# Four PSUM banks for the last MLP, and tasks that take turns where one MLP follows another

## The reference, cut to what matters

```
scores = q @ k.T / 8                        # 32 heads of 64 columns, 576 rows
p = exp(scores - max) where scores >= max - tau, else 0
x = (p / sum(p)) @ v                        # rows: (batch, 576), columns: 8 heads x 64

u = x + (x.T @ U @ V).T                     # mix over the 576 rows, rank 32
z = u + relu(u @ w_ch1) @ w_ch2             # MLP, 512 -> 2048 -> 512

logits = z @ w_gate; keep = sigmoid(z @ w_local) >= 0.5
e = previous row's expert where keep, else argmax(logits)
out = softmax(logits)[e] * (relu(z @ w1[e]) @ w2[e])     # 8 experts, 512 -> 1024 -> 512
```

## Time and profile before

| what | value |
|---|---|
| median of 3 runs | 1099.58 us (1099.11 to 1101.6) |
| the profiled execution's own time | 1100.43 us |
| its span, first to last instruction | 1098.7 us |
| TensorE busy | 1050.1 us, 96% |
| VectorE, ScalarE, GpSimd busy | 513.9, 469.9, 370.6 us |
| TensorE in the chain that ended last | 82% of the span |

### The profile page before, as it was taken

One profiled execution on the slowest core, in us unless ns is written; L12 is line 12 of the kernel. 1 busy time (PEld: TensorE's weight loads), 2 busy tenths in 40 slices (PEclk: granted clock), 3 DMA queues, 4 the chain that ended last, 5 costly groups with the idle time before them and its releaser, 6 DMA issues.

```text
span 1098.7 us, 20001 instructions
## 1 busy us (share of the span) xinstructions
PE 1050.1 (96%) x7142; PEld 920.0 (84%) x7142; DVE 513.9 (47%) x1022; ACT 469.9 (43%) x914; POOL 370.6 (34%) x341
## 2 busy tenths in 40 slices
PE   6999899999989999998999999899989999999997
PEld 5666799999769989986999997899978888888885
DVE  4675554445444444444454443322275543254642
ACT  5776543444454344445434433322214433244531
POOL 5454222624501553441064334068501111121111
PEclk9999999999999999999999999999999999999999
DMA  7887151535251542616052322432056444154621
GB/s 166 188 183 188 39 126 55 138 92 130 93 130 36 144 115 85 160 49 174 12 147 67 93 76 72 145 134 78 1 198 201 137 134 159 39 200 133 211 75 41
DMA packets 110729, 127.52 MB, mean 116 GB/s; under 512 B 67229, under 2 KB 67229, under 8 KB 110624
## 3 DMA queue, kind: packets, MB, share of 16 engines
q1 hardware_dynamic: 104480, 114.54, 36.7%
q0 software_dynamic: 3600, 11.01, 3.1%
q10 hardware_dynamic: 2544, 0.59, 0.2%
HBM read 88.16 MB, written 10.22 MB: 90 GB/s over the span
## 4 chain that ended last, share of the span: by engine, by line
PE 82%; SPq 6%; ACT 3%; DVE 3%; issue 3%; DMA 2%; POOL 0%; POOLq 0%; ACTq 0%; DVEq 0%
PE mlp_banks L697 19%; PE mlp_banks L689 18%; PE p_down L1387 11%; PE p_up L1387 11%; PE aux L647 6%; PE score_banks L623 5%; PE score_banks L630 5%; PE p_turn L1414 2%; DMA mlp_rows<-z_rows 1%; PE aux L590 1%; PE p_x L1381 1%; DVE stat L939 1%; PE mlp_banks L672 1%; SPq L291 1%; ACT u_hi L843 1%
## 5 line engine op out<-in xcount | busy, mean ns | idle before, releaser
L794 ACT ACTIVATE ex<-score_banks,stat 128x576 f32<-128x576 f32 x132 | 97.8, 741 | 178.0 <-DVE stat L939 178.0
L469 POOL CAST w_hi<-stage 128x1024 fp32r<-128x1024 f32 x64 | 66.6, 1040 | 288.1 <-PE mlp_banks L689 240.4
L689 PE MATMUL mlp_banks<-u_hi,w_hi 128*128 128x320 f32 (+1 forms) x512 | 157.0, 307 | 3.7 <-ACT u_hi L843 3.3
L697 PE MATMUL mlp_banks<-hid_hi,w_hi 128*128 128x320 f32 (+1 forms) x512 | 158.5, 309 | 0.9 <-DVE hid_lo L987 0.9
L948 DVE SCALAR_TENSOR_TENSOR ex<-score_banks,stat,ex 128x576 f32<-128x576 f32 x132 | 107.7, 816 | 107.0 <-ACT stat L798 105.7
L474 POOL TENSOR_TENSOR w_lo<-stage,w_hi 128x1024 fp32r<-128x1024 f32 (+1 forms) x70 | 154.1, 2203 | 4.8
L689 PE MATMUL mlp_banks<-u_hi,w_lo 128*128 128x320 f32 (+1 forms) x512 | 151.4, 296 | 0.0
L697 PE MATMUL mlp_banks<-hid_lo,w_hi 128*128 128x320 f32 (+1 forms) x512 | 151.3, 296 | 0.0
L697 PE MATMUL mlp_banks<-hid_hi,w_lo 128*128 128x320 f32 (+1 forms) x512 | 151.3, 296 | 0.0
L689 PE MATMUL mlp_banks<-u_lo,w_hi 128*128 128x320 f32 (+1 forms) x512 | 151.3, 295 | 0.0
L987 DVE SCALAR_TENSOR_TENSOR hid_lo<-mlp_banks,hid_hi 128x256 fp32r<-128x256 f32 (+1 forms) x128 | 58.4, 456 | 113.5 <-ACT hid_hi L845 112.8
(11 more groups left out here) (237 smaller groups left out, 1812.6 us busy)
## 6 DMA issues: line engine op xcount, KB each, us to landing
stage<-in_moe_w_ch SPq DMA_DIRECT2D x64, 512.0 KB, 3.7
w_raw<-in_moe_w SPq DMA_DIRECT2D x64, 512.0 KB, 5.1
q_tiles<-q_parts SPq DMA_DIRECT2D x30, 320.0 KB, 3.9
q_tiles<-q_parts SPq DMA_DIRECT2D x60, 160.0 KB, 4.2
k_tiles<-k_parts SPq DMA_DIRECT2D x60, 144.0 KB, 3.4
raw_q<-in_q SPq DMA_DIRECT2D x32, 128.0 KB, 3.1
raw_v<-in_v SPq DMA_DIRECT2D x32, 128.0 KB, 2.9
raw_k<-in_k SPq DMA_DIRECT2D x28, 128.0 KB, 2.7
```

Source lines behind the costliest of these rows:

```text
L469: nc.gpsimd.tensor_copy(w_hi[:, n % RING], stage[:, n % 2]).then_inc(w_upper, 1)
L689: last = nc.tensor.matmul(bank[:, 0:w], ch1(a, g, d, c), of[:, d, cols], start=(d == 0 and n == 0), stop=(d == KC - 1 and n == 2))
L697: last = nc.tensor.matmul(bank[:, 0:w], ch2(a, g, q, c), of[:, q, 0:w], start=(q == 0 and n == 0), stop=(q == QUARTER - 1 and n == 2))
L794: nc.scalar.activation(ex_of(n), score_of(n), ACT.Exp, bias=stat[:, n % 4, 0:1], scale=-1.0).then_inc(exp_done, 1)
```

## The change

`mlp_tasks` writes the list in another order. `banks_of_tasks` gives the tasks of the last batch, from `token_mix` to the last `logits`, four banks in turn: the two of `mlp_banks` and the first half of each of the two `score_banks`, which attention has left by then. Elsewhere a task's bank is t % 2 as before. `LEFT_BY[t]` is the task that used the bank before t; TensorE waits for its evictions.

- Start of batches 0 to 2: `mixed` of block 0 in turn with what batch b-1 left; then that rest in turn with the first `hidden` of block 0; then the first `channel` of block 0 in turn with `mixed` of block 1. In batch 0 nothing is left from before, so block 0's `mixed` and `hidden` stand alone.
- End of batches 0 and 1: `gate`, `logits` and the two `rows` of block 0 in turn with the last `hidden` of block 1. Block 1's last `channel`, `gate`, `logits` and `rows` are what is left to the next batch.
- Batch 2 to 3: `token_mix`, two `rows`, `mixed` of block 0, three `rows`, `mixed` of block 1.
- `tasks_by_step` has other counts of tasks per step; again 237 stand in attention's steps.
- `g4` has a buffer of its own, since `token_mix` now stands between `hidden` and `channel`. The last row of batch 2 is copied to `o_cols`, and doesn't wait for a store. `gate` of block 1 waits for the stores of the two rows of block 0 before it writes over `z_rows`. `logits` waits on TensorE for its own `gate`.
- The stationary side of the gate's products has 16 columns for 32; that of `rows` and `turn_out` for the last 64 rows has 64 for 128. Two clears at the start are gone.

The core of the diff:

```diff
 def mlp_tasks():
-    tasks = []
+    tasks, left = [], []
     for b in range(B):
+        def quarter(kind, k, r):
+            return [(b, kind, k, r, c) for c in range(KC)]
+
         rows = [(b, "rows", 0 if i < BLOCKS[0][1] else 1, i, 0) for i in range(NT)]
+        gate, logits = ([(b, kind, k, 0, 0) for k in range(2)] for kind in ("gate", "logits"))
         tasks.append((b, "token_mix", 0, 0, 0))
-        if b:
-            tasks += waiting
-        tasks += [(b, "mixed", k, 0, c) for k in range(2) for c in range(KC)]
+        if b < B - 1:
+            tasks += taking_turns(left[:KC], quarter("mixed", 0, 0))
+            tasks += taking_turns(left[KC:], quarter("hidden", 0, 0))
+            tasks += taking_turns(quarter("channel", 0, 0), quarter("mixed", 1, 0))
+        else:
+            tasks += left[:SPLIT_ROWS] + quarter("mixed", 0, 0) + left[SPLIT_ROWS:] + quarter("mixed", 1, 0) + quarter("hidden", 0, 0) + quarter("channel", 0, 0)
         for r in range(NQ):
             for k in range(2):
-                tasks += [(b, "hidden", k, r, q) for q in range(QUARTER)]
-                tasks += [(b, "channel", k, r, c) for c in range(KC)]
-        tasks += [(b, "gate", k, 0, 0) for k in range(2)]
-        tasks += [(b, "logits", k, 0, 0) for k in range(2)]
-        tasks += rows[:SPLIT_ROWS]
-        waiting = rows[SPLIT_ROWS:]
-    return tasks + waiting
+                if (r, k) not in ((0, 0), (NQ - 1, 1)):
+                    tasks += quarter("hidden", k, r) + quarter("channel", k, r)
+        if b < B - 2:
+            tasks += taking_turns([gate[0], logits[0]] + rows[:BLOCKS[0][1]], quarter("hidden", 1, NQ - 1))
+            left = quarter("channel", 1, NQ - 1) + [gate[1], logits[1]] + rows[BLOCKS[0][1]:]
+        else:
+            tasks += quarter("hidden", 1, NQ - 1) + quarter("channel", 1, NQ - 1) + gate + logits
+            left = rows
+    return tasks + left
...
+def banks_of_tasks():
+    first, last = INDEX[B - 1, "token_mix", 0, 0, 0], INDEX[B - 1, "logits", 1, 0, 0]
+    bank, user, left_by = [], {}, []
+    for t in range(len(TASKS)):
+        n = t - first
+        bank.append(t % 2 + (2 if first <= t <= last and n % 4 >= 2 else 0))
+        left_by.append(user.get(bank[t]))
+        user[bank[t]] = t
+    return bank, left_by
...
         if b == 1:
-            want = 0 if at == 0 else 1 if at == 1 else 3 if at in (6, 15, 17, 26) else 2
+            want = min(at, 2)
...
-            else:
-                pe.wait_ge(act_task, emptied(BY_ACT, t - 2))
-                pe.wait_ge(dve_task, emptied(BY_DVE, t - 2))
-            bank = mlp_banks[:, 512 * (t % 2):512 * (t % 2) + 512]
+            elif LEFT_BY[t] is not None:
+                pe.wait_ge(act_task, emptied(BY_ACT, LEFT_BY[t]))
+                pe.wait_ge(dve_task, emptied(BY_DVE, LEFT_BY[t]))
+            bank = task_bank(t)
...
             elif kind == "logits":
+                pe.wait_ge(act_task, emptied(BY_ACT, INDEX[b, "gate", k, 0, 0]))
...
+                if k == 1 and b < B - 2:
+                    act.wait_ge(rows_stored[0], 16 * (3 * b + 1))
+                    act.wait_ge(rows_stored[1], 16 * (2 * b + 1))
...
-                if b < B - 1 and stored:
+                if b < B - 1 and stored and (b, r) != (B - 2, NT - 1):
                     act.wait_ge(rows_stored[r % 2], 16 * stored)
```

More of the change, by code:

```diff
@@ L96, in tasks_by_step @@
     assert done == INDEX[B - 2, "channel", 1, NQ - 1, KC - 1] + 1
+    for want in (3, 1):
+        plan.append(list(range(done, done + want)))
+        done += want
     while done < len(TASKS):
@@ L202, in attention_and_mlp, with task_bank @@
     aux = ctx.enter_context(nc.psum_tensor("aux", [P, 1024], F32))
+    def task_bank(t):
+        n = BANK_OF[t]
+        return mlp_banks[:, 512 * n:512 * n + 512] if n < 2 else score_banks[:, n - 2, 0:512]
     def bank_of(n):
@@ L709, in task @@
                 for d in range(KC):
-                    last = nc.tensor.transpose(bank[:, d * P:(d + 1) * P], z_at(k, d, n * P, P), ident[:])
+                    last = nc.tensor.transpose(bank[0:ROWS[r], d * P:(d + 1) * P], z_at(k, d, n * P, ROWS[r]), ident[:])
             last.then_inc(task_done, 1)
```

39 lines of the change are left out of this document (23 added, 16 removed).

## The result

The changed kernel took 1093.2 us (median of 5 runs, 1091.9 to 1094.66) where the kernel before took 1099.58 (by now of 5 runs, 1099.11 to 1101.6): a ratio of 0.9932, with a 95% interval of 0.9922 to 0.9943. It is faster by 6.4 us by the medians; the ratio would be 7.5. The forecast was a gain of 15.9 and a range that ended at 1092, so the sign was right and both the time and the range were wrong.

The account below looks back on a forecast made before the run. TensorE, busy 96% of the span, was taken as the bound, so only its idle or slow-clock time could be won. 6.9 + 5.4 + 0.4 + 3.9 + 0.5 = 17.1 off 1100.43 gave 1083.3, against the median 1084.1; forecast 1083.7, range 1078.5 to 1092.

Parts of the forecast that it names:

- Part 1: The two borders inside attention: of 10.1 and 8.6 us lost, 3.2 stay at each, so gains of 6.9 and 5.4.
- Two kinds of stall stay: At each border inside attention, a step's chain (six times 0.45, 2.7 us) and waits inside `gate` and `logits` (0.5) stay.
- Clock: At the first border inside attention, TensorE ran mostly at 1.2 GHz after idling 1.69 us; counted as 1.6 us to win.
- Part 2: Start of the first MLP: two waits go, 1.3 us come back in steps 42 to 45; gain 0.4, between -2.5 and 1.7.
- Part 3: Last border: the first `hidden` starts at 694.9 for 698.8, a gain of 3.9 us, at worst 1.5.
- Part 4: Inside the last MLP and its end: a gain of 0.5 us in all (0 to 1), 0.4 at the end.
- Part 5: Small edits: nothing from 16 gate columns for 32 (-0.5 to +0.5 us), the 64-column transposes or the two dropped memsets.
- A: Rival: stalls only spread; 15 steps with one large task each lose 1.0 us, not 0.45; 1092 us, chance 19%.
- The forecast's own sign of being wrong: A gain under 9 us, with many waits of 1 us on the copies of turned scores, would make the forecast wrong.
- B: Rival: light steps borrow from fuller ones on both sides, 0.45 becomes 0.15 us; 5 us more, 1079, chance 11%.
- C: Rival: SP and GpSimd come late, the pair's stacking misses step 80; 2 x 11 us lost, 1106, chance 4%.
- D: Rival: the clock falls in the last MLP as TensorE goes round four banks; 1135 us if by half, chance 1%.

Follow-up runs that it names:

- e5: The changed kernel with VectorE evicting the first task before the mask of the next scores, in steps of three or more tasks: 1090.3 us, ratio 0.99.
- e4: The changed kernel with `mixed` of block 1 leading the first `channel` of block 0 in their turn: 1092.09 us, ratio 0.9926.
- e9: e6 with `row` 4 a step earlier (four tasks in step 79, two in 80, same at the second border): 1086.47 us, ratio 0.9874.
- e10: The kernel before with only VectorE's eviction of the first task moved in front of the mask, in steps of three or more tasks: 1097.92 us, ratio 0.9982.
- e1: The kernel before's task order in attention, with the changed last border, four banks in the last MLP and the small edits: 1095.27 us, ratio 0.9955.
- e3: The changed kernel with two banks in turn throughout, its task order kept: 1097.17 us, ratio 0.997.
- e7: The changed kernel with the last border in the order of the kernel before, the four banks kept: 1094.51 us, ratio 0.994.
- e6: The changed kernel with the edits of e4 and e5 together: 1087.94 us, ratio 0.988.

## Why the prediction was wrong

**Part 1 failed**, at its sentence "Two kinds of stall stay", and the 3.2 us a border that followed from it. The stalls that stay at the first border of the changed trace add up to some 6 to 7 us, an estimate: 4.9 us of idle time from 265 to 345 us, and some 0.2 more for each of nine waits, under a modelled end. Of the forecast's own two kinds, the scores' waits are 1.8, three of them where it had six; at `gate` and `logits` TensorE has no idle time at all. So what the forecast did count was if anything too dear. The rest is the three kinds that it left out, which it had at nothing: (c) at 299.43, 312.95 and 320.37, (d) at 343.80, (e) at 325.68. e5 took away the larger part of (c), e4 (d) and e9 (e), and they gave back 2.8, 3.0 and 0.8 us for both borders. By then 567.72 - 560.94 = 6.8 us of the shortfall were recovered by moving a few tasks and one eviction; against a forecast of 12.7 with the clock's share, about 2 stay open.

Why they were left out: I counted only TensorE's work and one chain in a step, and asked of each bank wait which engine the row names. I gave the small tasks better neighbours, and did not follow the third task's bank through VectorE's own order of instructions. The delay was there in the trace of before: an eviction ready at 317.4 starts on VectorE at 318.24. The Trainium skill's page "TensorE: Matmul & The Clock Gate" says in its section on the array's architectural detail that ScalarE's and VectorE's queues are strictly first in, first out; the traces agree, and e5 and e10 give the price, 2.8 and 2.3 us.

For one border alone the measure is clean: from step 72 to step 108 each kernel does 82 tasks, one whole MLP's worth of each kind. Before took 196.83 us from copy to copy (first fence), changed took 194.23 (second):

```profile
290.58 0.70 ACT L820 ACTIVATE et_first<-score_banks 128x640 f32<-128x640 f32 x1 [0.29 <-PE score_banks L630]
...
487.41 0.70 ACT L820 ACTIVATE et_first<-score_banks 128x640 f32<-128x640 f32 x1 [0.29 <-PE score_banks L630]
```

```profile
281.46 0.71 ACT L864 ACTIVATE et_first<-score_banks 128x640 f32<-128x640 f32 x1
...
475.69 0.71 ACT L864 ACTIVATE et_first<-score_banks 128x640 f32<-128x640 f32 x1
```

2.6 us less, 1.6 of it the clock's, as e1 shows, which has the order of before and no spell there (195.27): 1.0 for the reordering, where 5.3 were forecast beside the clock.

**Clock.** The 1.6 us were right as a price (196.83 - 195.27) and wrong as a fixed part of the border. Of 12 traces the spell fell at the first border in one, at the second in one (e1, where it cost less than 0.1), at 17 us in one, in the routing in six, and nowhere but at the span's very end in three. Its place is not free, though. In eight of the nine traces with a spell TensorE had stood idle for 1.3 to 1.9 us, and the granted clock fell 1.0 to 2.1 us after it resumed (before: 1.69 idle until 306.62, half clock from 307.7); the ninth, at 16.8 us, came behind two waits of 0.96 and 0.79. Such a wait can also pass without a fall (e1 at 307.53, and e10). The borders of the old order have waits of up to 1.85 us, those of the changed kernel none over 0.85 (1.38 in e4 and e6), and none of the nine traces with the new order had the spell at a border, against two of three with the old. That fits a change that takes away the occasion for it, but it is too few traces to say so.

**Part 2.** The start of the first MLP was forecast at a gain of 0.4 (its lower bound of -2.5 goes with 1.4 us for each of three steps; with 1.23, as it says, it would be -2.0). It can't be told apart from the second border with certainty, as step 72 ends with other tasks done in the two kernels. Together the two gained 3.9 - 2.6 = 1.3 us, where 5.8 were forecast. If the second border gained 1.0 as the first did, 0.3 is left for the start; by an estimate from the tasks' own durations 0.5 may as well be lost. It stays open within these.

**Part 3** was right: 4.2 us by the stage against 3.9. Its reasons were so only in part. It booked the gain to `token_mix` coming earlier and to the banks alike; e3 and e7 show that the banks bring 3.8 to 4.7 and the order at most 0.4.

**Part 4** expected 0.1 inside the last MLP and 0.4 at its end; both came out at zero (102.96 and 102.98; 25.69 and 25.75).

**Part 5** was right. The gate's products of 320 and 256 moving columns took 436 and 384 ns in the mean with 16 stationary columns in the changed kernel, and 441 and 391 with 32 in the kernel before.

**Rivals.** A's number was nearest, 1092 against 1093.2, but in good part by luck. It said that the stalls would only spread, each light step losing 1.0 us to its chain. Stalls did spread, but the scores waited only three times at a border, and most of the time went to banks and to `u_lo`. They were not the fixed price of a step either: e6 removes 6.0 us with the same work on all engines. The forecast's own sign of being wrong, a gain under 9 us with many waits of 1 us on the copies of turned scores, came in its first half alone. B's mechanism did not come. C is disproved: no scores waited for `q_tiles` or `k_tiles` at a border. D is disproved: the last MLP took 102.97 to 102.99 us in all eight traces with four banks, at clock 1.00. The Trainium skill's rule on going round banks (page "TensorE: Matmul & The Clock Gate", section "A second HAM failure mode: psum-queue depth-cycling") names short idle times between groups of products; TensorE had none inside this MLP, and four banks in turn brought neither idle time nor a lower clock, so how the clock answers such idle times was not tried here.

## What to carry to other kernels

When tasks are reordered to fill a tensor engine, follow each bank through the evicting engines' own order of instructions: an eviction behind an operation that waits for something else can cost as much as a bad order of tasks (2.3 us against 2.4 here), and moving it is an edit of three lines. A task that reads the newest eviction wants another task between, and a third task in a step wants the first one's bank emptied early or another bank; four banks for two brought some 4 of the 8.0 us by the traces. Before crediting a stall's removal with a clock spell, look for that spell in a second trace of the same kernel.

## What the runs showed that I had not expected

The spell of half clock, some 3.4 us long (6.8 in one trace), moves between runs of the same program: none in the changed kernel's first trace, at 816.0 us in its second. It costs 1.6 us where TensorE is full, less than 0.1 where it fills a wait that is there anyway, and 1.5 to 2.4 in the routing.

An idle gap of 1.7 us with the same tasks on both sides was followed by half clock in one trace and not in two others (e1 at 307.53, e10 at 305.35). What decides it was not tried.

A wait can be put down to the wrong engine where two evictions end close together: 299.43 names ScalarE's `u_hi` and was VectorE's add to z. Changing the order on the engine that the row did not name made it vanish.
